# Scores of two attentions in a fused fp32 kernel on one Trainium2 core: two products a tile in place of three, with a row addition behind them

## What is computed

```python
def sm_attn(qq, kk, vv):                       # batch 8, heads 8, seq 576, head_dim 64
    s = scale * np.matmul(qq, kk.transpose(0, 1, 3, 2))
    a = np.exp(s - np.max(s, axis=-1, keepdims=True))
    a = a / (np.sum(a, axis=-1, keepdims=True) + 1e-09)
    return np.matmul(a, vv)
p_packed = sm_attn(p, k, v)                    # p: 32 packed queries a head
out = sm_attn(q, p_packed, p_packed)
x = out.transpose(0, 2, 1, 3).reshape(4608, 512)
h = x @ w_in                                   # 512 x 2048
g = np.maximum(h, 0.0) + alpha * np.minimum(h, 0.0)
y = g @ w_out                                  # 2048 x 512
g2 = y @ w_gate                                # 512 x 1536, then w_out 1536 x 512
return (g2 / (1 + np.exp(-g2)) * (y @ w_val)) @ w_out2
```

## Time and profile before

| | us |
|---|---|
| runs, median of 3 | 1555.27 |
| runs, lowest to highest | 1554.94 to 1558.4 |
| profiled execution, its time | 1558.1 |
| profiled execution, its span | 1556.3 |
| TensorE matmul busy | 1548.7 |
| VectorE busy | 1110.5 |
| ScalarE busy | 708.1 |
| GpSimd busy | 176.7 |

### The profile page before, as it was taken

The page is one execution under the profiler, slowest core; times in us unless marked ns, Lnnn a source line. Parts: engine busy times, 40 slices in busy tenths (PEclk is TensorE's granted clock), DMA queues, the critical chain, the costliest instruction groups (busy, mean ns, idle before and its releaser), DMA issues.

```text
span 1556.3 us, 24850 instructions
## 1 busy us (share of the span) xinstructions
PE 1548.7 (100%) x9328; PEld 1435.6 (92%) x9328; DVE 1110.5 (71%) x1956; ACT 708.1 (45%) x1427; POOL 176.7 (11%) x194
## 2 busy tenths in 40 slices
PE   9999999999999999999999999999999999999999
PEld 6999999999999999999988888888888889999999
DVE  5565669877988779888755686557765685677666
ACT  4565567555765567655522252124422251234223
POOL 2654341000000010023200000000000000000000
PEclk9999999999999999999999999999999999999999
DMA  7443323442544345358466666676676668877866
GB/s 269 131 131 120 91 85 113 137 129 87 166 130 136 113 165 169 102 198 296 161 238 226 217 210 194 228 255 204 176 243 224 216 203 261 306 266 247 285 232 195
DMA packets 134503, 294.07 MB, mean 189 GB/s; under 512 B 13472, under 2 KB 44208, under 8 KB 134384
## 3 DMA queue, kind: packets, MB, share of 16 engines
q1 hardware_dynamic: 122400, 249.74, 49.7%
q0 software_dynamic: 11840, 42.48, 7.1%
q10 hardware_dynamic: 144, 0.26, 0.0%
HBM read 240.53 MB, written 51.90 MB: 188 GB/s over the span
## 4 chain that ended last, share of the span: by engine, by line
PE 96%; DVE 3%; DMA 1%; ACT 0%; issue 0%; DVEq 0%; ACTq 0%
PE acc L1070 14%; PE h L846 10%; PE h L848 10%; PE h L847 10%; PE side L846 9%; PE side L847 9%; PE side L848 9%; PE acc L1074 7%; PE acc L846 5%; PE acc L848 5%; PE acc L847 5%; DVE mixed L1536 1%; PE side L1004 1%; DVE piece L1536 1%; PE side L941 0%; DMA wring<-d_scratch 0%
## 5 line engine op out<-in xcount | busy, mean ns | idle before, releaser
L1070 PE MATMUL acc<-g,w 128*128 128x288 f32 x1792 | 272.8, 294 | 0.0
L1070 PEld LDWEIGHTS acc<-g,w 128*128 128x128 f32 x1792 | 248.9, 188 | 0.0
L1419 ACT ACTIVATE rows_b<-side 128x512 f32<-128x512 f32 (+1 forms) x60 | 33.4, 556 | 285.6 <-PE side L848 285.6
L1211 ACT ACTIVATE g<-floats 128x288 fp32r<-128x288 f32 x192 | 85.4, 445 | 165.0 <-DVE floats L1760 118.3
L1074 PE MATMUL acc<-g,w 128*128 128x288 f32 x896 | 156.2, 296 | 0.0
L846 PE MATMUL h<-attn,mixed 128*128 128x288 f32 x512 | 155.4, 303 | 0.5 <-DVE g L1536 0.5
L848 PE MATMUL h<-attn,mixed 128*128 128x288 f32 x512 | 151.1, 295 | 0.0
L847 PE MATMUL h<-attn,mixed 128*128 128x288 f32 x512 | 151.0, 295 | 0.0
L1074 PEld LDWEIGHTS acc<-g,w 128*128 128x128 f32 x896 | 131.2, 188 | 0.0
L1211 ACT ACTIVATE piece<-floats 128x512 fp32r<-128x512 f32 (+2 forms) x217 | 128.5, 616 | 3.2 <-PE side L848 2.9
L1536 DVE TENSOR_TENSOR g<-floats,g 128x288 fp32r<-128x288 f32 x192 | 87.3, 455 | 48.3 <-ACT g L1211 47.0
(11 more groups left out here) (324 smaller groups left out, 3934.8 us busy)
## 6 DMA issues: line engine op xcount, KB each, us to landing
ring<-w_scratch SPq DMA_DIRECT2D x90, 512.0 KB, 4.4
wring<-d_scratch SPq DMA_DIRECT2D x157, 256.0 KB, 2.9
ring_c<-w_scratch SPq DMA_DIRECT2D x60, 512.0 KB, 4.1
w_scratch<-piece POOLq DMA_DIRECT2D x36, 512.0 KB, 3.9
floats<-w_in SPq DMA_DIRECT2D x64, 256.0 KB, 3.1
ring_b<-w_scratch SPq DMA_DIRECT2D x30, 512.0 KB, 4.9
ring<-d_scratch SPq DMA_DIRECT2D x46, 256.0 KB, 2.9
d_scratch<-piece POOLq DMA_DIRECT2D x42, 256.0 KB, 3.5
```

What stands on the lines that cost most here:

```text
L1070: pe.matmul(acc[:, m, 0:CH], w2[:, j, x, m * P:(m + 1) * P], g[:, s % 2, 0, :], start=False, stop=False)
L1211: return nc.scalar.activation(dst, src, ACT.Copy, **kw)
```

## The change

For batches 1 to 7 both kinds of scores are formed piece by piece. In `pP` and `packT` the high half of the weights for the second product now holds, in the 64 columns that were empty for a pair of heads, the low part of the same heads. A piece of k or q then takes two products a tile: these filled weights times the high part of the piece, and the plain high weights times its low part. The high x high and high x low rows of the scores stand on 64 partitions of the bank, the low x high rows on the other 64. ScalarE copies the latter into `s1` or `attnF` at the place of the former (`low1`, `low2`), and VectorE adds the former from the bank (`join1`, `join2`); these steps are in the new list `JOIN`, which comes between `FRONT` and `MID`. A score step is 4 matmuls and has one piece; there are four a batch in the first attention and four in the second. The next user of the banks waits for the addition (`joined`). `max1`, `exp1` and `turn2` read the added rows in SBUF. Steps move: `max1`, `exp1`, `rec` by one slot; second scores' later steps by one, some `norm2` by several; the second piece of `scores2` stands in the next slot, or in slot 34, 47 or 56 for some; the mixes of batches 2 and 3 start one slot later; one piece a slot is split where two were.

The diff, cut to its core (semaphore names, the dispatch of the new steps and most of the table of slots are left out):

```diff
--- before
+++ after
@@ -99,8 +100,10 @@
 
 def _first_attention(b, at, turn=6):
     for half in range(2):
-        s = at + 3 * half
-        FRONT[s].append(("scores1", b, half))
+        for i in range(2):
+            s = at + 3 * half + i
+            FRONT[s].append(("scores1", b, half, i))
+            JOIN[s].append(("join1", b, half, i))
         BACK[s].append(("max1", b, half))
         MID[s + 1].append(("exp1", b, half))
         BACK[s + 1].append(("rec", b, half))
...
@@ -917,18 +948,16 @@
                     pe.matmul(hb[1][:, :], g_[:, 0:P], g_[:, P:P + 512], start=True, stop=True)
 
             def scores1(e):
-                _, b, half = e
+                _, b, half, i = e
                 once.wait_ge(p_split, b)
                 side_clear(e)
+                p = ("k", b, 2 * half + i)
+                piece_ready(p)
+                k = piece(p)
                 for c in range(2):
-                    for i in range(2):
-                        p = ("k", b, 2 * half + i)
-                        piece_ready(p)
-                        k = piece(p)
-                        mm = product(scores[:, c, :], hl(lambda x: pP[:, x, half, i, :]),
-                                     hl(lambda x: k[:, x, c * CH:(c + 1) * CH]), i == 0, i == 1)
-                        if c == 1 and i == 0:
-                            mm.then_inc(piece_left, 1)
+                    at = slice(c * CH, (c + 1) * CH)
+                    pe.matmul(scores[:, c, :], pP[:, 1, half, i, :], k[:, 0, at], start=True, stop=False)
+                    mm = pe.matmul(scores[:, c, :], pP[:, 0, half, i, :], k[:, 1, at], start=False, stop=True)
                 mm.then_inc(scores1_done, 1)
 
             def turn(e):
...
@@ -967,26 +996,23 @@
                 mm.then_inc(packT_done, 1)
 
             def scores2(e):
-                _, b, c = e
+                _, b, c, half = e
                 side_clear(e)
                 if b == 0:
                     once.wait_ge(q0_landed[c], 32)
-                    for half in range(2):
+                    for h in range(2):
                         for i in range(2):
-                            mm = pe.matmul(scores[:, half, :], packT0[:, half, i, :], q0[c][:, half, i, :],
+                            mm = pe.matmul(scores[:, h, :], packT0[:, h, i, :], q0[c][:, h, i, :],
                                            start=i == 0, stop=i == 1)
                     mm.then_inc(scores2_done, 1)
                     return
                 once.wait_ge(packT_split, b)
-                for half in range(2):
-                    p = ("q", b, c, half)
-                    piece_ready(p)
-                    q = piece(p).rearrange("p x (i n) -> p x i n", i=2)
-                    for i in range(2):
-                        mm = product(scores[:, half, :], hl(lambda x: packT[:, x, half, i, :]),
-                                     hl(lambda x: q[:, x, i, :]), i == 0, i == 1)
-                    if half == 0:
-                        mm.then_inc(piece_left, 1)
+                p = ("q", b, c, half)
+                piece_ready(p)
+                q = piece(p).rearrange("p x (i n) -> p x i n", i=2)
+                for i in range(2):
+                    pe.matmul(scores[:, i, :], packT[:, 1, half, i, :], q[:, 0, i, :], start=True, stop=False)
+                    mm = pe.matmul(scores[:, i, :], packT[:, 0, half, i, :], q[:, 1, i, :], start=False, stop=True)
                 mm.then_inc(scores2_done, 1)
 
             def mix_a(e):
...
@@ -1291,24 +1317,30 @@
                 ins.then_inc(spread_ready, 1)
 
             def split_p(b):
-                once.wait_ge(scores1_done, 2 * (b - 1))
+                if b > 1:
+                    once.wait_ge(scores1_done, scored(b - 1, 1, 1))
                 once.wait_ge(p_landed, 16 * b + 16)
-                copy(pP[:, 0, :, :, :], pRaw, scale=SCALE).then_inc(p_high, 1)
-
-            def exp1(e):
-                _, b, half = e
-                once.wait_ge(max1_ready, NTH[e] + 1)
+                copy(p_alone, pRaw, scale=SCALE).then_inc(p_high, 1)
+                copy(by_heads(p_both, b), by_heads(pRaw, b), scale=SCALE).then_inc(p_high, 1)
+
+            def low1(e):
+                _, b, half, i = e
+                once.wait_ge(scores1_done, scored(b, half, i))
                 if b == 1:
                     once.wait_ge(mix_done, 2 * KD)
-                    once.wait_ge(rec1_ready, 2)
                 else:
                     once.wait_ge(turned, ST * (b - 1))
-                    once.wait_ge(rec_ready, 2 * (b - 1))
                 beside = [j for j in range(before(e, "sums") // 2) if j not in STAGED]
                 if beside:
                     once.wait_ge(*low_of(("s", beside[-1], 1)))
-                nc.scalar.activation(s1[:, half, :].rearrange("p (c n) -> p c n", c=2), scores,
-                                     ACT.Exp, bias=nmax1[:, half:half + 1], accum_out=sum1[:, half:half + 1]
+                main, low = own(b, i), own(b, 1 - i)
+                copy(s1[main, half, :].rearrange("p (c n) -> p c n", c=2), scores[low, :, :]).then_inc(low_left, 1)
+
+            def exp1(e):
+                _, b, half = e
+                once.wait_ge(max1_ready, 2 + NTH[e] + 1)
+                once.wait_ge(rec1_ready if b == 1 else rec_ready, 2 if b == 1 else 2 * (b - 1))
+                nc.scalar.activation(s1[:, half, :], s1[:, half, :], ACT.Exp, bias=nmax1[:, half:half + 1], accum_out=sum1[:, half:half + 1]
                                      ).then_inc(exp1_done, 1)
 
             def turn(e):
...
@@ -1325,11 +1357,17 @@
                 once.wait_ge(packT_done, b)
                 if b == 1:
                     once.wait_ge(both_zeroed, 1)
-                blocks4 = side[:, 0, :].rearrange("p (h i n) -> p h i n", h=2, i=2)
-                copy(packT[:, 0, :, :, :], side[:, 0, :])
+                copy(pack_alone, side[:, 0, :])
+                copy(by_heads(pack_both, b), by_heads(side[:, 0, :], b))
+                copy(by_heads(both_high, b), by_heads(side[:, 0, :], b)).then_inc(packT_high, 1)
+
+            def low2(e):
+                _, b, c, half = e
+                once.wait_ge(scores2_done, NTH["scores2", b, c, half] + 1)
+                once.wait_ge(attn_split, 2 * (b - 1) + c + 1)
                 for i in range(2):
-                    ins = copy(both[:, 0, :, i, own(b, i)], blocks4[:, :, i, own(b, i)])
-                ins.then_inc(packT_high, 1)
+                    copy(attnF[own(b, i), c, half * CH:(half + 1) * CH], scores[own(b, 1 - i), i, :]
+                         ).then_inc(low_left, 1)
 
             def exp2(e):
                 once.wait_ge(sub2_done, NTH[e] + 1)
...
@@ -1569,15 +1611,26 @@
                 nc.vector.tensor_tensor(s4_, a12, s2_, ALU.subtract).then_inc(sums_step, 1)
 
             def split_p(b):
-                once.wait_ge(p_high, b)
-                nc.vector.scalar_tensor_tensor(
-                    out=pP[:, 1, :, :, :], in0=pRaw.rearrange("p (h i n) -> p h i n", h=2, i=2), scalar=SCALE,
-                    in1=pP[:, 0, :, :, :].bitcast(F32), op0=ALU.mult, op1=ALU.subtract).then_inc(p_split, 1)
+                once.wait_ge(p_high, 2 * b)
+                for half in range(2):
+                    at = slice(256 * half, 256 * half + 256)
+                    ins = nc.vector.scalar_tensor_tensor(
+                        out=by_heads(p_both[:, at], b, False), in0=by_heads(pRaw[:, at], b), scalar=SCALE,
+                        in1=by_heads(p_alone[:, at], b).bitcast(F32), op0=ALU.mult, op1=ALU.subtract)
+                ins.then_inc(p_split, 1)
+
+            def join1(e):
+                _, b, half, i = e
+                once.wait_ge(scores1_done, scored(b, half, i))
+                main = own(b, i)
+                once.wait_ge(low_left, lows_by(e))
+                into = s1[main, half, :].rearrange("p (c n) -> p c n", c=2)
+                nc.vector.tensor_tensor(into, scores[main, :, :], into, ALU.add).then_inc(joined, 1)
 
             def max1(e):
                 _, b, half = e
-                once.wait_ge(scores1_done, NTH[e] + 1)
-                nc.vector.tensor_reduce(nmax1[:, half:half + 1], scores, AX.XY, ALU.max,
+                once.wait_ge(joined, joined_by(("join1", b, half, 1)))
+                nc.vector.tensor_reduce(nmax1[:, half:half + 1], s1[:, half, :], AX.X, ALU.max,
                                         negate=True).then_inc(max1_ready, 1)
 
             def rec1_(e):
...
@@ -1678,22 +1731,30 @@
                                                    ).then_inc(turn_split, 1)
 
             def packedT(b):
-                blocks4 = side[:, 0, :].rearrange("p (h i n) -> p h i n", h=2, i=2)
                 once.wait_ge(packT_high, b)
-                subtract(packT[:, 1, :, :, :], blocks4, packT[:, 0, :, :, :])
+                subtract(by_heads(pack_both, b, False), by_heads(side[:, 0, :], b), by_heads(pack_alone, b))
```

(25 more changed lines are left out.)

75 lines of the change are left out of this document (52 added, 23 removed).

## The result

| | before | after |
|---|---|---|
| time, median | 1556.26 us (1554.94 to 1558.4) | 1595.87 us (1594.7 to 1597.36) |
| profiled execution | 1558.1 us, span 1556.3 | 1594.7 us, span 1592.9 |

The ratio is 1.0257, with a 95% interval of 1.0244 to 1.027. The forecast was 1583 us, with a range of 1561 to 1602. The direction and the mechanism held. The size was 12.9 us short.

What follows compares the result with a forecast made beforehand. TensorE, busy 1548.7 of 1556.3 us, was taken as the bound. Profiled 1558.1 - 14.9 saved + 42.5 of new waits = 1585.7, with the median 2.8 below: 1583 us, range 1561 to 1602.

Steps and rivals of the forecast that it cites:

- the mechanism: At reused score banks TensorE waits for VectorE's add, so VectorE's lag, free before, becomes TensorE's wait; +42.5 us in all.
- The saving: Batches 1 to 7: 112 score matmuls go, 0.133 us each, -14.9 us of TensorE time, all on the path.
- The new operations: VectorE's 28 adds of 64x576 and 56 of 64x288, 48 us less about 7; ScalarE's copies 0.66 and 0.4 us each.
- The stretch worked out: Batch 4, slots 83 to 88, lag followed slot by slot: TensorE waits of 1.6, 1.4, 2.9 and 1.8 us, sum 7.7.
- The 1.4 in slot 86: TensorE's wait for the g low that slot 86 reads: it ends at 6.2 us and is due at 4.8.
- The 1.8 at the transpose of slot 88: Transposes for the packed product are due 0.80 us into slot 88; late max and exp make TensorE wait 1.8 us.
- The sum: Batch 4's waits 9.5 us, batch 6 9.5, batch 5 6.5, batch 7 9, batches 1 to 3 8: +42.5 us.
- (1): Rival, chance 0.10: VectorE enters slots with an add at a lag under 1.5 us; -14.9 + 7, giving 1547 us.
- (2): Rival, chance 0.08: about even, 1555 us, if backlogs of slots 84 and 105 are half of those worked out.
- (3): Rival, chance 0.05: TensorE falls to 1.2 GHz after each of some ten long waits: +24 us, 1607 us.
- (4): Rival, chance 0.07: the ledger is too kind, with pieces or ScalarE late as well; 1602 us and more.
- The tests named: First 780 us: score-front waits for adds 20+ us, exp at turns about 8, VectorE over 90% near 300 and 490.

## Why the prediction came out as it did

**The saving** was right in kind and size, and hardly arrived. Busy time was to fall by some 15 us. In the changed kernel it fell by 0.8 only: matmuls at half the clock are busy 8.5 us longer, and with each wait a record stands whole where in a row it overlaps the next by 0.16 us. In the kernel with copies, adds and other work cut, with no fall, it fell by 14.2.

**The new operations** were costed well from rows of other shapes. The 576 add takes 0.67 us on the lower half (301.91 to 302.58) and 0.79 on the upper (305.26 to 306.05), and the instruction ahead of the latter takes 0.43 in place of 0.37: 0.67 and 0.85 against the forecast's 0.68 and 0.88. By the rule of the Trainium skill (VectorE: DVE Perf Modes, Two Vector instructions with no wait between them) the upper ones are held, and the 0.18 us agree. Two 288 adds take 0.94 against 0.92 (359.30 to 360.24):

```profile
359.30 0.91 DVE L1744 TENSOR_TENSOR floats<-side,floats 64x288 f32<-64x288 f32 x2
360.24 0.76 DVE L1578 TENSOR_TENSOR piece<-floats,piece 128x576 fp32r<-128x576 f32 x1
```

**The stretch worked out**, slots 83 to 88, was to grow by 6.6 us (7.7 of waits less 8 matmuls) and grew by 8.1 (17.7 to 25.8). Slot 84 of VectorE was to take 6.5 and took 6.63. The waits: 1.6 forecast and 1.88 measured at slot 84's front, 2.9 and 2.93 at slot 87's (by the slots' starts 2.05 and 3.13). The 1.4 in slot 86 isn't there, because the clock had fallen in slot 84 and TensorE came 1.6 us later; without a fall, 0.68 us of it shows at h. The 1.8 at the transpose of slot 88 shows as 0.47, again since the clock had fallen, and as 1.89 where it had not. So the total comes near partly by luck: 2.7 us of waits that the forecast had are not there, and the two falls, which it had not, lengthen slots 84 and 87 by 1.6 and 1.5. Slots 84 and 85 were to take over 7 us and took 6.93 (302.71 to 309.64), a near miss for the same reason.

**The sum** by stretches, from the starts of the slots in both timelines (us, after less before):

| slots | forecast | measured |
|---|---|---|
| 74 to 96, batch 4 | 9.5 - 2.1 = 7.4 | +7.6 |
| 96 to 116, batch 5 | 6.5 - 2.1 = 4.4 | +6.1 |
| 138 to 160, batch 6 | 9.5 - 2.1 = 7.4 | +8.8 |
| 160 to 180, batch 7 | 9 - 2.1 = 6.9 | +8.4 |
| 2 to 74 and 202 to 238 | 8 - 6.4 = 1.6 | +7.1 |
| all | +27.7 | +38.0 |

The term that was sized worst is the last row: batches 1 to 3, where I set 8 us by a glance at the few long waits. The terms named there do not even add up to it: 1.5 + 1 + 1.2 + 3 + 1.5, with 1 to 1.5 for batch 7's last scores, are 9.2 to 9.7. There slots 4 to 13 grew by 1.8 and slots 56 to 74 by 3.7. In the latter slots 59 and 60 grew by 1.8. The mix steps that move by one slot I had costed at nothing, because their readers are two slots away; but the last one now stands in slot 72, VectorE reads it only from 272.07 us on, behind four weight sums and a low part, and the piece in slot 74's front waits for that:

```profile
PE side L1014 <- DVE mixed L1578: 1.2, 1, 1.2
```

Over half of the miss (5.5 of 10.3) lies in that row, and nearly all the rest in 1 to 2 us for each of batches 5 to 7. That is 10.3 us between two profiles. The start ran 2.0 us shorter by itself (slot 2 began at 34.7 and not 36.7), and what lies behind slot 238 is 0.6 longer. The other 4 us of the 12.9 are the choice of the execution: the forecast took off 2.8 us, by which before's profiled one lies above the median of three runs, and after's lies 1.2 below its own median.

**The rivals.** (1) and (2), the adds fit or the waits just eat the saving, are out: about even is what the run had in which copies, adds and VectorE's other work were all cut. (3), the waits cost clock, came half true. The falls came, five of them, and behind long waits as it said. They cost 1.5 us, where ten were priced at 24. I had priced a fall at TensorE's lost speed, as if TensorE set the time there; but these five are followed by another wait for VectorE or ScalarE, which takes the lost speed back. Where none follows, a fall costs most of it, as the last section shows. (4), pieces or ScalarE late as well, didn't show: no transfer is in the list of waits of the first 780 us, and a piece only with 0.4 us, as before (0.45).

**The tests named.** Waits at the fronts for adds 22.9 us (20 and more forecast), VectorE 9.77 and 9.58 of 10 us busy from 300 and from 490 (over 90%), the second half unchanged. Waits at h and y for g and its float 4.6 us. At the transposes 3.0 us for exp, where 8 was said, and 3.2 for an add; with the five falls gone the former are nearer (7.6 us in the run with idle matmuls in eight places).

## What to carry to other kernels

An engine that is late and waited for by nobody holds a credit; before a change puts one of its results on the path (here: a bank that is reused one slot later), read its lag at each of those places, since the lag is part of the price. Here the 40 us of loss hold some 20 for the lag and some 20 for the new copies and adds (8 of them for the adds), and most of the 14.9 us saved still did not arrive when both were cut. Saved TensorE time counts only where TensorE sets the time, and the same is true of lost clock. To tell price from backlog, cut other work of the late engine in both kernels: the same 35 us were worth 0 in one and 20 in the other.

## What the runs showed of the hardware that I had not expected

The same wait doesn't always bring the same clock. In front of the transpose of slot 48, TensorE stood for 3.15 us in the changed kernel and for 3.16 in the first kernel with idle matmuls, and the program up to there is the same. The clock stayed in the first and fell in the second (a matmul of 288 columns in 0.29 and in 0.44 us; windows of 4 us):

```profile
192.45 0.41 PE L970 MATMUL side<-floats 128*128 128x128 f32 x2 [3.15 <-DVE floats L1744]
...
193.23 0.30 PE L878 MATMUL acc<-g,w 128*128 128x288 f32 x1
```
```profile
194.34 0.66 PE L1008 MATMUL side<-floats 128*128 128x128 f32 x2 [3.16 <-DVE floats L1823]
...
195.28 0.44 PE L895 MATMUL acc<-g,w 128*128 128x288 f32 x1
```
```profile
190.00:194.00 4.00, 1.18 (x9) 0.95 (x8) 3.87 (x10) 2.80 (x8) 1.93 (x2) 0.94 0.41 131
194.00:198.00 4.00, 3.66 (x16) 3.69 (x17) 2.19 (x6) 0.93 (x4) 1.26 (x1) 0.50 0.47 154
198.00:202.00 4.00, 4.00 (x25) 4.00 (x25) 2.62 (x4) 2.10 (x6) 1.28 (x1) 0.71 0.05 17
```

The missing clock is 4 x (0.06 + 0.50 + 0.29) = 3.4 us there, twice that of the others. And here it cost: slots 42 to 56 took 48.5 us with the fall and 45.8 in the kernel with idle matmuls in all thirteen places, 2.7 us more. The second fall of that execution, 1.7 us from 326.6 on, cost too: it began right behind the wait of 1.89 us at slot 88's transposes, and slots 83 to 90 took 29.6 us and 28.1 in the kernel without falls. Behind slots 48 and 88 no long wait follows, and TensorE sets the time; between slots 84 and 88 waits follow, and they take the lost speed back. So the price of a fall depends on what stands behind it.

These falls do not explain the medians of the two kernels (1598.5 and 1595.8). The profiled execution is the slowest of the four, 1599.9 us with a mean granted clock of 0.997; the other three show 0.999, which is room for one fall of 1.7 us and not for these two, and take 1596.8 to 1598.9. So at least 1.0 of the 2.7 us between the medians stays unexplained. What decides whether a wait brings the fall stays open as well.
